# The first product of a second MLP by seven block products instead of eight, in a fused attention and two-MLP kernel

## The reference

```python
rms = sqrt(mean(x * x, -1) + 1e-6);  xn = x / rms * rms_g
g = xn @ w_gate                          # 512 x 1536
x2 = (g * sigmoid(g) * (xn @ w_val)) @ w_out
h = x2 @ w_in                            # 512 x 2048
out = (h * sigmoid(1.702 * h)) @ w_out2  # 2048 x 512
```

## Time and profile before

| | us |
|---|---|
| median of 3 runs | 924.08 (923.71 to 924.46) |
| the profiled execution | 924.33 |
| its span, first to last instruction | 922.5 |
| PE busy in it | 910.3 |
| DVE busy | 370.4 |
| ACT busy | 306.1 |
| POOL busy | 105.1 |

### The profile page before, as it was taken

One profiled execution on the slowest core, in us unless ns is written; L12 is line 12 of the kernel. 1 busy time (PEld: TensorE's weight loads), 2 busy tenths in 40 slices (PEclk: granted clock), 3 DMA queues, 4 the chain that ended last, 5 costly groups with the idle time before them and its releaser, 6 DMA issues.

```text
span 922.5 us, 13523 instructions
## 1 busy us (share of the span) xinstructions
PE 910.3 (99%) x5324; PEld 763.2 (83%) x5324; DVE 370.4 (40%) x878; ACT 306.1 (33%) x736; POOL 105.1 (11%) x146
## 2 busy tenths in 40 slices
PE   8799999999999999999999999999999999999998
PEld 7799888888888888888888888888888888888897
DVE  6896533334343344423354542242224223322332
ACT  5666333343332433423111322232223223222232
POOL 6234001220021201112122200000000000000000
PEclk9999999999999999999999999999999999999999
DMA  7672111201121101203132230020002000200100
GB/s 253 205 218 79 49 49 50 72 32 41 49 67 55 46 27 55 67 1 104 57 109 97 69 114 1 1 91 1 1 1 92 0 1 1 69 1 0 43 4 24
DMA packets 33680, 52.92 MB, mean 57 GB/s; under 512 B 3408, under 2 KB 14160, under 8 KB 33616
## 3 DMA queue, kind: packets, MB, share of 16 engines
q1 hardware_dynamic: 32208, 50.35, 17.2%
q10 hardware_dynamic: 1408, 1.70, 0.5%
HBM read 42.60 MB, written 9.44 MB: 56 GB/s over the span
## 4 chain that ended last, share of the span: by engine, by line
PE 94%; DVE 3%; ACT 1%; issue 1%; ACTq 0%; DVEq 0%
PE ps L540 22%; PE ps L541 22%; PE ps L542 22%; PE ps L694 7%; PE ps L695 7%; PE ps L696 7%; PE ps L525 2%; PE ps L497 2%; PE ps L511 1%; DVE w_all L947 1%; ACT prob L723 1%; PE ps L537 0%; DVE sig L991 0%; PE ps L617 0%; DVE prob L903 0%
## 5 line engine op out<-in xcount | busy, mean ns | idle before, releaser
L540 PE MATMUL ps<-x_hi,w_all 128*128 128x512 f32 (+1 forms) x800 | 298.9, 374 | 0.2 <-DVE x_lo L928 0.2
L542 PE MATMUL ps<-x_lo,w_all 128*128 128x512 f32 (+1 forms) x800 | 294.7, 368 | 0.0
L541 PE MATMUL ps<-x_hi,w_all 128*128 128x512 f32 (+1 forms) x800 | 294.6, 368 | 0.0
L540 PEld LDWEIGHTS ps<-x_hi,w_all 128*128 128x128 f32 x800 | 150.7, 188 | 29.9 <-issue 3.9
L541 PEld LDWEIGHTS ps<-x_hi,w_all 128*128 128x128 f32 x800 | 150.9, 189 | 25.7 <-issue 1.0
L542 PEld LDWEIGHTS ps<-x_lo,w_all 128*128 128x128 f32 x800 | 150.8, 188 | 25.3
L1063 DVE TENSOR_TENSOR hid<-ps,sig 128x512 f32<-128x512 f32 (+1 forms) x80 | 51.0, 638 | 207.7 <-ACT sig L856 207.5
L856 ACT ACTIVATE sig<-ps 128x512 f32<-128x512 f32 (+1 forms) x80 | 44.4, 555 | 215.5 <-PE ps L542 215.5
L695 PE MATMUL ps<-w_all,h_hi 128*128 128x512 f32 x288 | 112.3, 390 | 0.0
L694 PE MATMUL ps<-w_all,h_hi 128*128 128x512 f32 x288 | 112.3, 390 | 0.0
L696 PE MATMUL ps<-w_all,h_lo 128*128 128x512 f32 x288 | 112.1, 389 | 0.0
(11 more groups left out here) (96 smaller groups left out, 830.1 us busy)
## 6 DMA issues: line engine op xcount, KB each, us to landing
wstage<-in_w_a SPq DMA_DIRECT2D x36, 256.0 KB, 3.3
vwin<-in_v_win SPq DMA_DIRECT2D x32, 256.0 KB, 3.8
wstage<-in_w_b SPq DMA_DIRECT2D x32, 256.0 KB, 3.0
kwin<-in_k_t SPq DMA_DIRECT2D x32, 160.0 KB, 3.4
out_dram<-late SPq DMA_DIRECT2D x18, 256.0 KB, 2.1
qtok<-in_q_t SPq DMA_DIRECT2D x34, 128.0 KB, 2.5
xT<-x_scratch SPq DMA_DIRECT2D x4, 1024.0 KB, 5.3
x_scratch<-wstage SPq DMA_DIRECT2D x3, 1024.0 KB, 4.2
```

The lines of the kernel that those rows point to most:

```text
L540: pe.matmul(out_, w[:, 0, cols], xh, start=first, stop=False, **flags)
L541: pe.matmul(out_, w[:, 1, cols], xh, start=False, stop=False, **flags)
L542: return pe.matmul(out_, w[:, 0, cols], xl, start=False, stop=last, **flags)
```

## The change

The second MLP's first product is made by Strassen's algorithm in Winograd's form. A pair of chunks (256 hidden columns) times a tile, now of 768 tokens, is cut into 2 x 2 blocks: w_in into chunk x half of d, x2 into half of d x 384 tokens. Seven products of such blocks take the place of eight; each is two blocks of d, three passes, six matmuls of 384 columns. With S and T for sums of blocks:

S1 = A21 + A22, S2 = S1 - A11, S3 = A11 - A21, S4 = A12 - S2; T1 = B12 - B11, T2 = B22 - T1, T3 = B22 - B12, T4 = B21 - T2; P1 = A11 B11, P2 = A12 B21, P3 = S4 B22, P4 = A22 T4, P5 = S1 T1, P6 = S2 T2, P7 = S3 T3; C11 = P1 + P2, u2 = P1 + P6, u3 = u2 + P7, C21 = u3 + P4, C22 = u3 + P5, C12 = u2 + P5 + P3.

PE adds in the bank where it can: P2 onto P1 in bank 6; P7 onto P6, then P4 onto both in bank 7; P3 onto P5 in bank 6. DVE adds the rest (`make_u`, `make_c`) with a copy of P1 that ACT makes (`save_s1`). There are 3 tiles x 8 pairs = 24 pairs. The weights no longer stay: each tile reads them again, a pair's w_in (512 KB) and w_out (512 KB) in turn into three places; POOL makes the sums S for each pair (`combine_w2`, four operations) and T for each tile (`combine_x2`, `last_x2_sum`); ACT casts, DVE makes the low parts of seven blocks of weights per pair and, one block per pair, of the next tile's seven blocks of x2. Six y banks take 768 tokens. The output products of the pair before run in two blocks of six units (three matmuls each), behind P7 and behind P3. At the start the pair 0 is interleaved with the last two projections of A.

The core of the diff:

```diff
-    TILES_B = ((0, 512), (512, 512), (1024, 512), (1536, 512), (2048, 256))
-    NA, NB = len(TILES_A), len(TILES_B)
+    NA = len(TILES_A)
+    NB = 3
...
+            def load_w2(k):
+                g, m = (k // 2 - 1, 1) if k % 2 == 0 and k > 0 else ((k + 1) // 2, 0)
+                f = 2 * (g % PB)
+                if k >= RAWS:
+                    sp.wait_ge(w2_split, pieces_before(k - RAWS + 1))
+                sp.dma_start(raw2(k).rearrange("p (f n) -> p f n", f=2),
...
             def load_x2(j):
+                wait(sp, xcB_lo, COMBOS * j)
+                sp.dma_start(x2raw[:, :, :], x2[:, :, j * TB:(j + 1) * TB].rearrange("c p t -> p c t")
+                             ).then_inc(x2_loaded, 16)
...
+            for k in range(RAWS):
+                load_w2(k)
+            load_w2(in_unit(2))
+            load_x2(1)
             store_x2(NA - 1)
+            for g in range(1, NP):
+                load_w2(out_unit(g))
+                if g + 2 < NP:
+                    load_w2(in_unit(g + 2))
+                if g == PB:
+                    sp.wait_ge(x2_stored, 16 * NA)
+                    load_x2(2)
+                if g % PB == 2 and g > PB:
+                    store_out(g // PB - 1)
+            store_out(NB - 1)
...
+            def combine_w2(g):
...
+                if g > 0:
+                    pool.wait_ge(w2_split, pieces_before(in_unit(g - 1)) + IN_PIECES)
+                pool.wait_ge(w2_loaded[in_unit(g) % RAWS], raw2_loaded(in_unit(g)))
+                nc.gpsimd.tensor_tensor(s1_, a21, a22, ALU.add).then_inc(w2_combined, 1)
+                nc.gpsimd.tensor_tensor(s3_, a11, a21, ALU.subtract).then_inc(w2_combined, 1)
...
+            combine_x2(0)
+            last_x2_sum(0)
+            combine_w2(0)
+            combine_w2(1)
+            for g in range(NP):
+                if g + 2 < NP:
+                    combine_w2(g + 2)
+                if g % PB == 0 and g // PB + 1 < NB:
+                    combine_x2(g // PB + 1)
+                if g % PB == 5 and g // PB + 1 < NB:
+                    last_x2_sum(g // PB + 1)
...
+            def product_1(g):
+                pe.wait_ge(w2_split, pieces_before(in_unit(g)) + IN_PIECES)
+                if g % PB == 0:
+                    pe.wait_ge(xcB_lo, COMBOS * (g // PB + 1))
...
+                    pe.wait_ge(cB_made, 3 * g)
+                product(g, P1, BANK_A, True)
...
+            product_1(0)
+            product_6(0)
+            project_A(NA - 1, CA - 2)
+            product_2(0)
+            project_A(NA - 1, CA - 1, range(0, 1))
+            product_7(0)
+            project_A(NA - 1, CA - 1, range(1, DC))
+            product_5(0)
+            product_4(0)
+            product_3(0)
+            for g in range(1, NP):
+                product_1(g)
+                product_6(g)
+                product_2(g)
+                product_7(g)
+                out_B(g - 1, range(0, 6))
+                product_5(g)
+                product_4(g)
+                product_3(g)
+                out_B(g - 1, range(6, 12))
+            out_B(NP - 1, range(0, 2 * SUB))
```

The order of ACT and of DVE in a pair:

```diff
+            for g in range(NP):
+                j, p = divmod(g, PB)
+                save_s1(g)
+                if g > 0 and g + 1 < NP:
+                    w2in_hi(g + 1, range(IN_PIECES))
+                sigmoid_B(g, C11)
+                w2out_hi(g, 0)
+                hid_hi_B(g, C11)
+                w2out_hi(g, 1)
+                if g == 0:
+                    evacuate_A(NA - 1)
+                if p > 0 and j + 1 < NB:
+                    xcB_hi_block(j + 1, p - 1)
+                sigmoid_B(g, C22)
+                hid_hi_B(g, C22)
+                sigmoid_B(g, C21)
+                hid_hi_B(g, C21)
+                sigmoid_B(g, C12)
+                if p == 0 and j > 0:
+                    evacuate_y(j - 1)
+                hid_hi_B(g, C12)
...
+            for g in range(NP):
+                j, p = divmod(g, PB)
+                make_u(g, u2, P6)
+                if g + 1 < NP:
+                    w2in_lo(g + 1, range(IN_PIECES))
+                hidden_B(g, C11)
+                w2out_lo(g, 0)
+                make_u(g, u3, P7)
+                hid_lo_B(g, C11)
+                w2out_lo(g, 1)
+                if g == 0:
+                    evacuate_A(NA - 1)
+                if p > 0 and j + 1 < NB:
+                    xcB_lo_block(j + 1, p - 1)
+                make_c(g, C22)
+                hidden_B(g, C22)
+                make_c(g, C21)
+                hid_lo_B(g, C22)
+                hidden_B(g, C21)
+                hid_lo_B(g, C21)
+                make_c(g, C12)
+                hidden_B(g, C12)
+                if p == 0 and j > 0:
+                    evacuate_y(j - 1)
+                hid_lo_B(g, C12)
```

More of the change, by code:

```diff
@@ new lines, in fused_attention_mlps, with xcB, xcB_last_slot, w2in_last_slot @@
+        C11, C22, C21, C12 = range(4)
+        SIDES = {P1: (A11, B11), P6: (S2, T2), P2: (A12, B21), P7: (S3, T3),
+                 P5: (S1, T1), P4: (A22, T4), P3: (S4, B22)}
+        IN_PIECES, OUT_PIECES = 4, 2
+        def xcB(j):
+            return xcB_odd if j % 2 else xcB_even
+        def xcB_last_slot(k):
+            return k // 2
+        def w2in_last_slot(g):
+            return 4 + g % 2
+        def hB_of(g, chunk, part):
+            return hB[:, g % 2, part, chunk, :]
+        def block_of(g, which):
+            chunk, half = {C11: (0, 0), C12: (0, 1), C21: (1, 0), C22: (1, 1)}[which]
+            return [hB[:, g % 2, part, chunk, half * HB:(half + 1) * HB] for part in range(2)]
@@ L601, in project_A @@
                     pe.wait_ge(hidA_made, 2)
-                for j in range(DC):
+                for j in parts:
                     if c == 0:
@@ new lines, in product_3, with out_B @@
+            def product_3(g):
+                pe.wait_ge(cB_made, 3 * g + 1)
+                product(g, P3, BANK_A, False)
+            def out_B(g, units):
+                if g < 0:
+                    return
+                j, p = divmod(g, PB)
+                for i in units:
+                    half, chunk, s = i // SUB, (i // (SUB // 2) + i // SUB) % 2, i % (SUB // 2) + i // SUB * (SUB // 2)
+                    first = chunk == half
+                    pe.wait_ge(w2_split, pieces_before(out_unit(g)) + chunk + 1)
+                    pe.wait_ge(hidB_lo, 4 * g + 1 + {(0, 0): C11, (0, 1): C12, (1, 0): C21, (1, 1): C22}[chunk, half])
+                    if p == 0 and first:
@@ L693, in out_B @@
+                    y = ps[:, s, :]
                     rows = slice(s * P, (s + 1) * P)
[L694 to L698 removed]
@@ L699, in out_B @@
-                ins.then_inc(projB_done, 1)
-            pe.wait_ge(hidA_made, CA * NA)
-            for j in range(NB):
-                for f in range(CB + LAG):
-                    if f < CB:
-                        in_B(j, f)
-                    if f >= LAG:
-                        out_B(j, f - LAG)
+                    last = p == PB - 1 and not first
+                    h, w = hB_of(g, chunk, 0), w2out[:, g % 2]
+                    pe.matmul(y, h[:, rows], w[:, 0, chunk, :], start=(p == 0 and first), stop=False)
```

509 lines of the change are left out of this document (300 added, 209 removed).

## The result

The changed kernel takes **919.38 us** (median of 5 runs, 918.79 to 919.88), the kernel before 924.08 (5 runs, 923.71 to 924.46). The ratio is 0.9948 (95% interval 0.9935 to 0.996): 4.7 us faster. The forecast was 10.6 us faster. The profiled execution has a span of 917.7 us; before it was 922.5.

The account below looks back on a forecast made before the run. TensorE, busy 99%, was taken as the bound. Matmuls -22.5 us, then +1.5, 0.8, 3.2, 2.2, 1.6, 2.3 and 0.2 for stalls and clock gave -10.7 from 924.33: 913.6, put at 913.5; range 905 to 921.5.

Parts of the forecast that it names:

- the second rival: Handovers before P3, P2 and P7 each 0.1 us beyond their narrow margins, in 23 pairs: 6.9 us, result 920.5; chance 0.22.
- P1(0): Seam between the MLPs: pair 0's P1 waits for the seventh block of x2, 0.8 us.
- the narrow margins of 0.07 and 0.15: Steady pairs: slack before P3 (0.07 us), P2 (0.15) and P7 (0.07), expected to hold.
- The three other rivals: Queues fit with room, 906 (0.17); DVE becomes the bound through POOL, 937 (0.07); shorter slot not brought, 923 (0.04).
- the third: DVE loses all of POOL's adds; pairs with an x2 block stall 1.3 us, others 0.37: 937; chance 0.07.
- P3(0): Seam, pair 0's P3: no wait forecast, 0 us.
- P1(1): Seam, pair 1's P1: 3.2 us waiting for C12's sum plus 2.2 for POOL's x2 sums blocking DVE.
- The clock: Behind the seam's idle stretch the granted clock falls, costing 1.6 us (bounds 0 and 1.6).
- Pairs with an x2 block: POOL's weight sums hold DVE up before C22's sum: 0.1 us in each of 14 pairs, 1.5 us.
- Tile changes: Pair 8, next x2 combination and y's copies: 2.3 us; pair 16, copies alone: 0.2.

Follow-up runs that it names:

- experiment 5: Changed kernel with the last three projections of A moved behind P3 of pair 0 and the copies of A's sums moved later: 922.61 us.
- experiment 8: Changed kernel with projections behind P3 of pair 0, x2 low part late, x2 sums spread and fewer waits in the output blocks, together: 911.74 us.
- experiment 1: Changed kernel without POOL's sums of x2 for the second and third tile: 912.98 us.
- experiment 3: Changed kernel with 24 more matmuls of 384 columns, read by nothing, between P3(0) and P1(1): 917.22 us.
- experiment 2: Changed kernel without POOL's sums of the weights from the third pair on: 916.11 us.
- experiment 6: Changed kernel with DVE's x2 low part moved behind the low part of C12, except in a tile's last pair: 916.61 us.
- experiment 11: Changed kernel with the first block of six output units split, three before P7 and three behind it: 925.07 us.
- experiment 4: Changed kernel with the two waits of an output unit only at the first of three units: 918.92 us.
- experiment 7: Changed kernel with POOL's x2 sums spread over pairs 0, 1, 2 and 5 of a tile, each after the pair's last low part: 916.43 us.
- experiment 9: All the moves together, with the weight loads for pair 1's output and pair 3's input issued before the store of A's last tile: 908.36 us.

## Why the prediction was right, and where its size was not

**Right.** The direction, the gain in matmul time and the kinds of loss. 22.5 us for 384-column slots at 0.1732: found are 0.1733, and the account closes on 22.5 to within 0.2. That 919.4 lies inside the range is luck in part: the upper end was drawn over the second rival, whose waits are not there. P1(0) waits 0.8 for the seventh block. DVE operations of 384 columns take 0.56, casts 0.51, sigmoids 0.49 to 0.53. PE doesn't wait for P2 and P7 in steady pairs, so the narrow margins of 0.07 and 0.15 hold, and the second rival, whose 920.5 is near the result, names the wrong cause. Weight loads cost nothing while their order stands, and experiments 5 and 8 show the price when one comes late. The three other rivals are false: the queues do block; a pair with an x2 block stalls at P3 alone, as the third said, but by 0.21 and not 1.3; and the slot is what the fit said.

The step that failed is the sum of stalls: 11.8 us forecast, 18.3 found. By its terms:

- **P3(0), priced at nothing, 1.3 us found.** I put POOL's sums of x2 at 530 to 536 across C22 and C21, and looked for no step ahead of the sum of C22. What they met first was the output weight's low part (2.36 us in place of 0.68), with the first MLP's two copies in the same queue behind it. Experiment 1, without the sums, has no such stall.
- **P1(1), 5.4 forecast, 4.5 found.** 3.2 us for the C chain alone is right (3.2 in experiment 1). The blocking adds 1.2 there instead of 2.2, since part of it had already come at P3(0). Together the two places are 5.8 against 5.4, which is near by chance: one of the steps that were held was not in the forecast.
- **The clock, 1.6 forecast, 2.7 found**, above the 1.6 that was given as the upper bound. I took the length of the half clock from the earlier trace rows. Here it began while PE stood, within 537 to 539, and lasted over 18 slots, 17 of them of 0.32 us instead of 0.173, to 545.3. Experiment 3 shows the cost alone: 2.7 for these slots in its trace, 2.4 over the whole trace and 2.2 in its median.
- **Pairs with an x2 block, 14 x 0.1 forecast, 13 x 0.21 found.** POOL's 256-column operations with two inputs take 0.74 to 1.20 us, not the 0.61 of the earlier trace rows, so the last still runs when DVE reaches the x2 low part, which takes 1.49 for 0.95. Experiments 2 and 6 take away the one or the other, and both end the stall. DVE has no idle time left before the sum of C22 in such pairs, where the forecast had a little. That it is not POOL's sums of x2 is experiment 1's finding. The Trainium skill (SBUF — State Buffer, Who interferes with whom) has a DVE instruction with two SBUF inputs and a GpSimd instruction that reads SBUF exclude each other. These rows agree: sums with a PSUM input kept 0.54 to 0.56 us beside POOL, and only the others grew. I had its rule as a bound and gave POOL a loss of less than half by the earlier trace rows; neither the whole nor that part was right everywhere.
- **Tile changes, 2.5 forecast, 2.8 found**: at pair 8, 2.0 before P1 where 1.3 was forecast, and 0.8 before P2 and P7 where y's copies were to cost 1.0; nothing at pair 16 instead of 0.2. That the sums agree is partly chance: in experiment 1 the copies stand and the whole 2.8 is gone, so without the blocking they cost nothing.
- **Changes of width, not priced, 3.2 us of the last row's 3.5.** I read the price of a slot inside long stretches of one width, where the excess is nil. The kernel before shows the effect behind those rows: its last tile's six 512-column slots from 878.35, behind 256-column ones, take 1.39 us to 879.74 instead of 1.36. Experiment 11 adds two changes and gets 0.07 a pair; 2 and 4 leave POOL and the waits out of it. Other operands and another bank alone don't make it either: the kernel before changes both 106 times at one width and loses nothing behind it. So it goes with the width; why a changed width costs this stays open.

Experiments 5 to 9 also show that the terms at the seam don't add. The fall of the clock, the wait at P1(1) and that at P3(0) hang on the same few DVE steps, and a better order takes most of all three at once.

## What to carry to other kernels

When an algorithm saves TensorE work in a kernel that TensorE bounds, the gain is sure and the price lies in the helpers: here 4.7 of the saved 22.5 us reached the end of the kernel, and 16.1 once the other engines' steps were in another order. Keep GpSimd's SBUF sums away in time from VectorE's steps with two SBUF inputs on the tight chain; give TensorE work, even useless work, across an idle stretch of some 3 us; and before a step is moved, look in SyncE's queue for a store that waits for it and for the loads behind that store. Price matmul slots in the mixture in which they will run, not in the middle of long stretches.

## What the runs showed of the hardware that was not expected

- A matmul stream is slightly wide for the first six to nine slots behind a change of width, 0.041 us per change from 384 to 512 columns and 0.025 back. A change of operands and bank at one width cost nothing.
- The half clock cost more the second time. PE idled 4.4 us and then did 5.9 us of unbroken matmuls at 1.2 GHz. After 3.2 us of idle time (experiment 1) the clock fell as well, to 0.57 and 0.58 over 539 to 543, which is 3.4 us at half: as much as the 0.59 over 4 us in the earlier trace rows. A wait of 1.2 us (experiment 9) lowered nothing.
- The same idle stretch does not always lower the clock. The stretch of the earlier trace rows lies in the attention, which the change leaves alone, and in the changed kernel's trace PE works as little in it (0.77 of 3.5 us), but the clock behind it stays at 1.00:

```profile
38.00:42.00 4.00, 3.20 (x52) 2.96 (x55) 3.97 (x9) 2.54 (x6) 0.00 (x0) 1.00 0.53 162
```

- A VectorE operation of 512 columns with two SBUF inputs that takes 0.68 us alone took 2.36 beside a GpSimd sum of 768 columns (2.19) and ended 0.5 behind it: the short one can be held for nearly the whole of the long one.
- A remedy that only adds work won: 4.2 us of matmuls that nobody reads made the kernel 2.2 us faster. The two moves of experiments 6 and 7 won more on their own, 2.8 and 2.9.
